# Attention scores as three split products, and a reordered Fourier tail, in a four-batch mixer kernel

## What is computed

```
state = alpha[t] * state + k[t] v[t]^T ; y[t] = q[t] state      # attention, per batch and head
u = x + real(fft(fft(x, tokens), columns))                       # x is y, heads side by side
un = normalise(u) ; x2 = u + relu(un @ w_ch1) @ w_ch2             # first MLP
z = relu(x2^T @ w_tok1) @ w_tok2 ; u2 = x2 + z^T                  # token mix
out = u2 + relu(u2 @ w2_ch1) @ w2_ch2                             # second MLP
```

## Time and profile before

| | |
|---|---|
| three runs, median | 893.28 us |
| three runs, lowest and highest | 890.87 and 893.49 us |
| profiled execution, its own time | 890.61 us |
| its span on the core | 888.8 us |
| PE busy | 875.4 us (98%) |
| DVE busy | 437.6 us (49%) |
| ACT busy | 326.6 us (37%) |
| POOL busy | 189.8 us (21%) |
| granted TensorE clock | 1.00 in every stretch asked for |

### The profile page before, as it was taken

One profiled execution on the slowest core, in us unless ns is written; L12 is line 12 of the kernel. 1 busy time (PEld: TensorE's weight loads), 2 busy tenths in 40 slices (PEclk: granted clock), 3 DMA queues, 4 the chain that ended last, 5 costly groups with the idle time before them and its releaser, 6 DMA issues.

```text
span 888.8 us, 14640 instructions
## 1 busy us (share of the span) xinstructions
PE 875.4 (98%) x5386; PEld 846.9 (95%) x5386; DVE 437.6 (49%) x1078; ACT 326.6 (37%) x843; POOL 189.8 (21%) x321
## 2 busy tenths in 40 slices
PE   8999999999999999999999999999999999999998
PEld 6789889999999999999999999999999999999998
DVE  6778867567766577675542253222432142214121
ACT  2865674335654246653224332211221122112111
POOL 4733444023332024330113402000200020002000
PEclk9999999999999999999999999999999999999999
DMA  9961220040220412200072011000100010000000
GB/s 213 327 185 33 61 61 28 1 121 28 68 55 28 106 41 62 61 22 7 1 251 88 27 54 55 1 28 27 53 0 27 27 53 0 27 27 0 0 27 27
DMA packets 15002, 51.23 MB, mean 58 GB/s; under 512 B 1489, under 2 KB 6385, under 8 KB 13009
## 3 DMA queue, kind: packets, MB, share of 16 engines
q1 hardware_dynamic: 14368, 47.35, 17.9%
q0 software_dynamic: 576, 3.15, 0.9%
HBM read 41.07 MB, written 9.44 MB: 57 GB/s over the span
## 4 chain that ended last, share of the span: by engine, by line
PE 87%; DVE 4%; ACT 3%; DMA 2%; issue 2%; SPq 1%; DVEq 0%; POOL 0%; ACTq 0%
PE bank L1427 13%; PE bank L1429 13%; PE bank L1428 13%; PE pair L1427 12%; PE pair L1428 12%; PE pair L1429 12%; PE pair L1445 3%; PE bank L1464 3%; DMA qkap<-qka 2%; PE bank L1473 2%; PE pair L1454 1%; PE bank L1573 1%; ACT tested L731 1%; PE bank L1626 1%; PE bank L1434 1%
## 5 line engine op out<-in xcount | busy, mean ns | idle before, releaser
L1289 DVE SCALAR_TENSOR_TENSOR hl<-bank,hh 128x384 fp32r<-128x384 f32 x192 | 106.8, 556 | 332.7 <-ACT hh L825 332.5
L825 ACT ACTIVATE hh<-bank 128x384 fp32r<-128x384 f32 x192 | 94.3, 491 | 337.2 <-PE bank L1429 336.8
L1427 PE MATMUL bank<-nh,w1h 128*128 128x384 f32 x288 | 101.8, 353 | 0.2
L1427 PE MATMUL pair<-w2h,hh 128*128 128x384 f32 x288 | 101.2, 351 | 0.2 <-DVE u L1170 0.2
L1427 PE MATMUL bank<-u2h,w3h 128*128 128x384 f32 x288 | 97.0, 337 | 0.9 <-DVE u2l L1383 0.9
L1427 PE MATMUL pair<-w4h,hh 128*128 128x384 f32 x288 | 97.2, 338 | 0.0
L1428 PE MATMUL pair<-w4l,hh 128*128 128x384 f32 x288 | 97.0, 337 | 0.0
L1428 PE MATMUL pair<-w2l,hh 128*128 128x384 f32 x288 | 96.8, 336 | 0.0
L1429 PE MATMUL pair<-w2h,hl 128*128 128x384 f32 x288 | 96.8, 336 | 0.0
L1429 PE MATMUL bank<-nh,w1l 128*128 128x384 f32 x288 | 96.8, 336 | 0.0
L1428 PE MATMUL bank<-nl,w1h 128*128 128x384 f32 x288 | 96.8, 336 | 0.0
(11 more groups left out here) (201 smaller groups left out, 1838.0 us busy)
## 6 DMA issues: line engine op xcount, KB each, us to landing
qkap<-qka SPq DMA_DIRECT2D x15, 1011.5 KB, 7.6
vt<-v SPq DMA_DIRECT2D x16, 288.0 KB, 7.9
raw_a<-w_ch SPq DMA_DIRECT2D x6, 768.0 KB, 10.7
mid<-u SPq DMA_DIRECT2D x8, 576.0 KB, 2.8
raw_b<-w_ch SPq DMA_DIRECT2D x6, 768.0 KB, 6.3
out<-u SPq DMA_DIRECT2D x8, 576.0 KB, 2.8
xr<-mid SPq DMA_DIRECT2D x7, 576.0 KB, 3.8
raw_t<-w_tok SPq DMA_DIRECT2D x2, 768.0 KB, 6.0
```

The costliest lines, as they stand in the source:

```text
L825: act.activation(hh[:, s % 4, :], bank[s % 2][:, 0:HALF], ACT.Relu).then_inc(s_hhi, 1)
L1289: dve.scalar_tensor_tensor(out=hl[:, s % 4, :], in0=bank[s % 2][:, 0:HALF], scalar=0.0, in1=hh[:, s % 4, :].bitcast(F32), op0=ALU.max, op1 ...
L1427: pe.matmul(out_ap, wh, rh, start=first, stop=False)
```

## The change

1. **Scores of batches 1 to 3.** ACT makes three copies per step in place of two, all rounded to fp32r: the keys (`kh`) and the queries of each head (`qh`). POOL subtracts to get the low parts of the keys (`kl`) and of head 0's queries (`ql`), DVE those of head 1. PE then makes `three` products of 256 columns in place of one float32 product. The tiles lie over tiles of the tail, so POOL clears `ql` once per batch.
2. On POOL a visit is now: low parts of step k+2, decay of step k+2, `prep` of step k+3.
3. The two range tests of a unit go into two neighbouring visits.
4. In batch 0's tail ACT copies the flipped rows and the edge rows between its splits of `xf`, ahead of the splits of `g`.
5. In `fourier_v` DVE first forms the difference and the sum of `f2_u` and `f2_v`, and adds each to rows 0 and 1 with one operation per half, in place of adding the two terms one after the other. Counts and waits that hang on this are renumbered.

The core of the diff, in this order: POOL's visit and `split_low`; ACT's copies, range tests and its splits of `xf` in the tail; DVE's visit and `fourier_v`; PE's `attn_scores`.

```
     def visit(a, k):
+        split_low(a, k + 2)
+        decay(a, k + 2)
         prep(a, k + 3)
-        decay(a, k + 2)
...
+    def split_low(a, k):
+        if k < STEPS:
+            pool.wait_ge(s_sc, a * STEPS + k - 1)
+            pool.wait_ge(s_qz, 3 * ((a - 1) * STEPS + k) + 3)
+            if k == 0:
+                pool.wait_ge(s_clear, a)
+            pool.tensor_tensor(kl[0:PR, k % 2, :], k_of(a, k), kh[0:PR, k % 2, :].bitcast(F32), ALU.subtract
+                               ).then_inc(s_low[0], 1)
+            r = head_rows(0)
+            pool.tensor_tensor(ql[r, k % 2, 0, :], q_of(a, k, r), qh[r, k % 2, 0, :].bitcast(F32), ALU.subtract
+                               ).then_inc(s_low[0], 1)
...
-    def attn_qz(a, k, h):
+    def attn_high(a, k):
         if k < STEPS:
             act.wait_ge(s_qk, 2 * prepared(a, k))
             act.wait_ge(s_sc, a * STEPS + k - 1)
-            act.activation(qz[head_rows(h), k % 2, h, :], q_of(a, k, head_rows(h)), ACT.Copy).then_inc(s_qz, 1)
+            if k == 0:
+                act.wait_ge(s_uv, 4 * a)
+            act.activation(kh[0:PR, k % 2, :], k_of(a, k), ACT.Copy).then_inc(s_qz, 1)
+            for h in range(2):
+                act.activation(qh[head_rows(h), k % 2, h, :], q_of(a, k, head_rows(h)), ACT.Copy).then_inc(s_qz, 1)
...
-        if a and k > 0 and k % NC == 2 and k // NC + 1 < NU:
-            for i in range(2):
-                range_of(a, k // NC + 1, i)
+        if a and k > 0 and k % NC in (1, 2) and k // NC + 1 < NU:
+            range_of(a, k // NC + 1, k % NC - 1)
...
+            if a == 0 and i == 2:
+                copy_flipped(0)
+            if a == 0 and i == 3:
+                first_edge_rows()
...
         attn_state(a, k + 1)
         if a:
+            split_low(a, k + 2)
             prep(a, k + 3)
...
     def fourier_v(a):
+        dve.wait_ge(s_uv, a * 4 + 1)
+        for dst, op in ((diff, ALU.subtract), (total, ALU.add)):
+            dve.tensor_tensor(dst, u0, vs[:, 0, :], op).then_inc(s_diff, 1)
...
+        for t, src, left, right in ((0, x[:, 0], diff, total), (1, u[:, 1], total, diff)):
+            dve.tensor_tensor(u[:, t, 0:n], src[:, 0:n], left[:, 0:n], ALU.add).then_inc(s_ua, 1)
+            dve.tensor_tensor(u[:, t, n:DM], src[:, n:DM], right[:, n - 2:0:-1], ALU.add).then_inc(s_ua, 1)
...
-        pe.wait_ge(s_qz, 2 * ((a - 1) * STEPS + k) + 2)
-        return pe.matmul(score_bank(a, k)[:, 0:2 * P], k_of(a, k),
-                         qz[0:PR, k % 2, :, :].rearrange("p h t -> p (h t)"), start=True, stop=True)
+        for i in range(2):
+            pe.wait_ge(s_low[i], (2 - i) * ((a - 1) * STEPS + k + 1))
+        high, low = (q[0:PR, k % 2, :, :].rearrange("p h t -> p (h t)") for q in (qh, ql))
+        return three(score_bank(a, k)[:, 0:2 * P], kh[0:PR, k % 2, :], kl[0:PR, k % 2, :], high, low, True, True)
```

More of the change, by code:

```diff
@@ L127, in program @@
     alpha1 = sb("alpha1", [P, AW], o + S * 4)
+    ql = sb("ql", [P, 2, 2, P], o + XB, F32R)
+    kh = sb("kh", [P, 2, P], o + XB + 4 * P * 4, F32R)
+    assert XB + 6 * P * 4 <= 8 * GW * 4
     gh = sb("gh", [P, 4, GW], o, F32R); o += 4 * GW * 4
@@ L226, in program @@
               "at_ready", "state_ready", "visit_done", "x_ready"])
+    s_diff, s_clear = map(sem, ["difference_ready", "q_low_cleared"])
+    s_low = [sem(f"qk_low_ready_{n}") for n in ("pool", "dve")]
     s_dec = [sem(f"state_decayed{h}") for h in range(2)]
@@ L247, in program @@
               "u2_lo"])
-    UA = 10
+    UA = 12
     DVE_TILES = (0, 2, 3)
@@ L659, in _ @@
                     prep_q(a + 1, 0, 1)
+                    clear_low(a + 1)
             for i in range(2 * NW4):
@@ L735, in visit @@
             def visit(a, k):
-                for h in range(2 if a else 0):
-                    attn_qz(a, k + 2, h)
+                if a:
+                    attn_high(a, k + 2)
                 attn_krt(a, k + 2)
@@ L774, in copy_v @@
                 if j == 2:
-                    act.wait_ge(s_v0, a * 4 + 4)
+                    act.wait_ge(s_ua, a * UA + 4)
+                elif j == 1:
+                    act.wait_ge(s_diff, a * 2 + 2)
                 elif a:
                     act.wait_ge(s_pv, a * 8)
-                act.activation(vs[:, j % 2, :], v_bank(a, j)[:, 0:FW], ACT.Copy,
+                act.activation(vs[:, j // 2, :], v_bank(a, j)[:, 0:FW], ACT.Copy,
                                scale=col[:, 0:1] if j == 0 else 1.0).then_inc(s_vc, 1)
@@ L1064, in x_sum, with split_low @@
                                          (ALU.add, ALU.subtract)[part])
+            def split_low(a, k):
+                if k < STEPS:
+                    r = head_rows(1)
+                    dve.wait_ge(s_sc, a * STEPS + k - 1)
+                    dve.wait_ge(s_qz, 3 * ((a - 1) * STEPS + k) + 3)
+                    if k == 0:
+                        dve.wait_ge(s_clear, a)
+                    dve.tensor_tensor(ql[r, k % 2, 1, :], q_of(a, k, r), qh[r, k % 2, 1, :].bitcast(F32), ALU.subtract
+                                      ).then_inc(s_low[1], 1)
             def early_sum(a, part):
@@ L1149, in fourier_v @@
             def fourier_v(a):
+                n, u, u0 = DM // 2 + 1, us[a % 2], u_bank(a, 0)[:, 0:FW]
+                diff, total = vs[:, 1, :], both[:, :]
+                dve.wait_ge(s_vc, a * 3 + 1)
+                if a:
+                    dve.wait_ge(s_pv, a * 8)
+                dve.wait_ge(s_uv, a * 4 + 1)
+                for dst, op in ((diff, ALU.subtract), (total, ALU.add)):
+                    dve.tensor_tensor(dst, u0, vs[:, 0, :], op).then_inc(s_diff, 1)
+                dve.wait_ge(s_diff, 2 * a + 2)
                 dve.wait_ge(s_rows, a + 1)
[L1152 to L1155, removed]
+                for t, src, left, right in ((0, x[:, 0], diff, total), (1, u[:, 1], total, diff)):
+                    dve.tensor_tensor(u[:, t, 0:n], src[:, 0:n], left[:, 0:n], ALU.add).then_inc(s_ua, 1)
+                    dve.tensor_tensor(u[:, t, n:DM], src[:, n:DM], right[:, n - 2:0:-1], ALU.add).then_inc(s_ua, 1)
             def fourier_u(a, first, n, i):
@@ L1164, in fourier_u @@
                 if i == 0:
[L1165 to L1168, removed]
+                    dve.wait_ge(s_pv, a * 8 + 2 * (first + n - 2))
                     dve.wait_ge(s_uv, a * 4 + (1, 3, 4)[j])
@@ L1252, in tail @@
                     fourier_v(a)
-                    for i in range(2):
-                        fourier_u(a, 0, 2, i)
                 if h == MIDDLE_AT:
```

34 lines of the change are left out of this document (18 added, 16 removed).

## The result

The change took 926.07 us (median of four runs; three of them 925.95 to 926.19) against 893.06 us for the kernel before in the same measurement: a ratio of 1.0374, 95% interval 1.0356 to 1.0392. It is 33 us slower where 6.5 were forecast, and outside the range.

The account below looks back on a forecast made before the run. PE's time was taken as the bound (busy 119.90 of 120 us in batch 3). Batches 2 and 3 +6.8, batch 1 +1.1, batch 0's tail -1.4 make +6.5 on 893.28: 899.8 us, range 889 to 913.

Parts of the forecast that it names:

- the chain: Scores, batches 1 to 3: ACT copies, POOL's two subtractions, decay, two multiplications, copies again; 3.2 us against PE's 2.94.
- Products: PE's scores: three 256-column products cost .39 against .44, saving .05 a score, 3.6 us over 72 where PE sets pace.
- Rival 3: PE's scores get no cheaper, three weight loads take the saving, products .17 each; 902.1 us, chance .15.
- The loop's length: Time from one step's copies to the next's: summed to 3.10 us, taken as 3.2; 3.0 without decay.
- A subtraction is taken at the multiplication of the same 128 columns, .39: POOL's low keys and low queries were each priced at .39 us, from the multiplication's start-to-start time.
- I take their waits at nothing: Batches 2 and 3, eight visits behind pauses: no waits, at most .2 each (1.6); steps 7 to 15 gain .45.
- batch 1 at +1.1: Batch 1's 22 visits, without a pause: the loop makes 69.8 us for 68.71.
- up to 2 more if DVE, late, adds to the loop: Batch 1: DVE's wait for the copies delays work queued behind it, costing up to 2 us more.
- Rival 2: POOL and DVE take turns at the shared SBUF port, loop 3.6 us; +22, 915.4 us, chance .15.
- Rival 1: PE keeps the pace: a POOL subtraction costs about .2, loop 2.8 hides behind 2.94; -5.0, 888.3 us, chance .18.
- At nothing: Items priced at no cost: Fourier sums in batches 1 to 3, range tests, clearing of `ql`, with no DMA touched.
- The tail: Batch 0's tail: moving flips and edge rows ahead returns 1.4 of PE's 1.54 us idle (0 to 1.7).

Follow-up runs that it names:

- with the loop open: The change with low parts computed for steps 0 and 1 of each batch only, reused by the other steps; 889.48 us, ratio .9969 against the kernel before.
- the multiplications first: The change with POOL's multiplications and DVE's scans of step k+3 ahead of the subtractions of step k+2; 928.25 us, ratio 1.0399 against the kernel before.
- without_new_scores: The change with the scores left as in the kernel before, all else changed; 886.43 us, ratio .9937 against the kernel before.
- prepared_two_ahead: The change with scans and multiplications for step k+4 instead of k+3, both range tests in one visit again; 908.10 us, ratio 1.0182 against the kernel before.
- tests_in_one_visit: without_new_scores with both range tests of a unit in one visit again; 889.93 us, ratio .9977 against the kernel before.

## Why the prediction was wrong

The direction, the chain and the place of its last link were right. The size was not. By spans the change costs 35.5 us (the profiled execution of before was one of its shortest), and the forecast of 6.5 falls short by 29: 12.2 in batch 1, 16.2 in the visits of batches 2 and 3, .3 ahead of their first scores, .4 ahead of batch 1's.

- **Products: right.** .05 a score where PE sets the pace (.06 measured with the loop open). Rival 3 falls.
- **The loop's length: the subtraction was mis-sized.** "A subtraction is taken at the multiplication of the same 128 columns, .39": .53 and .56 were measured, and so 1.50 from the copies' end to the score (425.83 to 427.33) for .95. The multiplication of the queries that lent its price came behind DVE's scans; the subtractions lie beside DVE's subtraction and suffix scan. Beside the masking of scores, in an early visit of batch 3, the low keys take .47. The Trainium skill (SBUF — State Buffer, "Who interferes with whom") has the one that issues first keep the shared port, and the other fully blocked. Of the long pair POOL was the blocked one (1.47, ending at 432.20, .30 behind DVE's sum), though it began .14 earlier as the rows time it. The short pairs differ from the rule: both run at once, and the low keys grow by .1, DVE's suffix scan from .42 to .57.
- **Where the forecast failed: "I take their waits at nothing" behind the pauses, and batch 1 at +1.1 with "up to 2 more if DVE, late, adds to the loop".** +3.04 (for -.45) and +12.74 were measured. The steps right behind a pause lost nothing, as forecast (4.29 against 4.28 at step 8), but five of the visits that follow lost .34 to 1.03 each, where .2 was the most allowed. The stretches without a pause missed by less, 1.9 and 2.7 a batch. All these steps used one length of the loop, read from a visit with nothing else in it, and asked how much start a pause gives. But the loop passes through ACT, POOL and DVE in the order of their instructions, and what stands in those rows (sums, norms, weight splits, the hidden parts) is now inside the loop: 30 visits have 3.5 to 4.6. Before, with the same lumps in the rows, PE idled .1 us in 120 of batch 3. The evidence: with scans and multiplications two ahead, the last stretch is back at PE's pace with all the operations still there; with single links moved (three kernels), the next arm took over within some 5 us.
- **Rival 2, POOL and DVE in turns: a part.** The two subtractions are .31 longer than priced, most of the .37 by which a plain visit exceeds PE's 2.94: 38 visits by .37 make 14 us. In ten of the 30 longer visits, eight of them in batch 1, one of POOL's multiplications takes 1.04 to 1.49 beside a weight split or a sum of DVE (.92 to 1.05), 8.4 us in all over .44 each, and ACT's next copy starts within .04 of the end of POOL's queries; so these turns are part of the longer visits too. Ten such multiplications (1.04 to 1.14) stand in the kernel before, where PE's waits for POOL come to .9. Loops of 3.6 and more do not come in plain visits, and shorter operations without a shorter chain (the multiplications first, .473) won nothing. Whether the loop would fit PE's pace if the subtractions lay beside nothing was not tried.
- **Rival 1 falls:** no subtraction on POOL was near .2, and PE waits.
- **"At nothing": the range tests were wrong** (a gain of 3.5 us by the medians). The first scores of batches 2 and 3 come .95 late, forecast .80. The tail was right in kind: PE's 1.54 is gone.

What is not settled: how the rest of the gap divides between the late first steps, batch 1 and DVE's lumps, and among the lumps between their place in the order and POOL's turns with DVE; no kernel was tried that frees all of these.

## What to carry to other kernels

A new chain through several engines is not priced by its length beside the period it must fit: with no slack, every lump on any of those engines' rows is added, so list the visits in which one stands and price them, above all where a row of before shows an engine 80 of 120 us busy. If two arms of a loop are nearly equal, shortening one shows nothing; move the whole loop a step apart (work one more step ahead) before counting instructions. And try the side edits alone: here they held all the gain, and spreading two tests over two visits was worth about what the scores were to save (3.5 us by the medians, 3.6 forecast).

## What the chip did that I had not expected

A wait of PE can cost more than itself. With both range tests in one visit, PE waited 1.5 us ahead of step 11 of batch 1; in the windows from 112 us on the granted clock (the first number behind the counts) read:

```profile
112.00:115.00 3.00, 1.50 (x10) 1.16 (x10) 2.04 (x7) 2.37 (x7) 0.41 (x1) 1.00 0.00 0
115.00:118.00 3.00, 3.00 (x13) 3.00 (x13) 2.76 (x7) 1.74 (x5) 2.18 (x4) 0.52 0.00 0
118.00:122.00 4.00, 4.00 (x27) 3.87 (x26) 2.13 (x6) 1.89 (x7) 1.21 (x4) 0.93 0.26 53
```

.52, near the lower level of 1.2 GHz, for three microseconds, and step 12 took 4.28 in place of without_new_scores' 2.84. The profiled execution of prepared_two_ahead has it too: PE waited 1.77 ahead of step 10 of batch 3, and the windows from its end on read

```profile
373.70:376.90 3.20, 3.16 (x18) 3.19 (x19) 3.07 (x9) 2.34 (x7) 2.60 (x7) 0.76 0.02 5
376.90:380.00 3.10, 3.10 (x15) 3.10 (x14) 0.34 (x1) 0.04 (x1) 0.47 (x2) 0.70 0.00 0
```

with the 6.02 of step 11 inside. In batch 2 of the same execution the window behind the same wait stayed at 1.00, and the profiled execution of the kernel before had a wait of 1.47 with no drop. A drop like this would fit the spread of the runs of before that were taken beside the experiments, between 890.0 and 893.7: those up to 891.6 have a mean granted clock of 1.000, those above .995 to .998. The runs of tests_in_one_visit spread from 888.8 to 891.9 beside the .8 us of without_new_scores, which has no such wait. That the clock fell behind this wait in those runs isn't shown, since only one execution of each kernel was profiled.
